# Routing in two interleaved chains, its constants made earlier, and the sixth weight unit's second half loaded later

## The reference

```
1. attention with gates, a recurrence over 768 positions, for 4 batches x 8 heads of width 40:
   C = f*C + i*(v k^T);  y = sigmoid(o) * (C q) / max(|n q|, 1)
2. mixture of 8 experts:  logits = x @ w_gate;  e = argmax(logits)
   out[token] = softmax weight of e * (relu(x @ w1[e]) @ w2[e])
3. dense pair:  h = x @ w_in;  out = max(0.01 h, h) @ w_out
```

## Time and profile before

| | us |
|---|---|
| three runs | 809.02, 803.6, 808.95 |
| median | 808.95 |
| profiled execution, its own time | 808.7 |
| its span, first to last instruction | 807.0 |
| PE busy | 744.9 (92%) |
| DVE busy | 518.1 (64%) |
| ACT busy | 415.4 (51%) |
| POOL busy | 192.6 (24%) |

### The profile page before, as it was taken

One profiled execution on the slowest core, in us unless ns is written; L12 is line 12 of the kernel. 1 busy time (PEld: TensorE's weight loads), 2 busy tenths in 40 slices (PEclk: granted clock), 3 DMA queues, 4 the chain that ended last, 5 costly groups with the idle time before them and its releaser, 6 DMA issues.

```text
span 807.0 us, 17962 instructions
## 1 busy us (share of the span) xinstructions
PE 744.9 (92%) x6435; PEld 551.7 (68%) x6436; DVE 518.1 (64%) x1346; ACT 415.4 (51%) x811; POOL 192.6 (24%) x286
## 2 busy tenths in 40 slices
PE   4899999995488999999999899999999999999994
PEld 3688888885277888888888655556566555565552
DVE  6769898897887457565687565465465455554441
ACT  4578777767753458455664233343433433434332
POOL 4477787874221101111100000020100100100101
PEclk9999999998699999999999999999999999999998
DMA  6879979660527965887220000000000000000000
GB/s 195 221 232 294 326 234 340 184 203 26 176 69 266 358 219 198 262 317 256 84 83 1 2 2 1 0 34 1 25 9 2 32 0 0 32 0 0 34 1 32
DMA packets 39517, 95.87 MB, mean 119 GB/s; under 512 B 7150, under 2 KB 19630, under 8 KB 39438
## 3 DMA queue, kind: packets, MB, share of 16 engines
q1 hardware_dynamic: 31010, 66.33, 26.3%
q10 hardware_dynamic: 5788, 19.47, 6.7%
q0 software_dynamic: 2640, 9.01, 3.4%
HBM read 70.92 MB, written 23.89 MB: 117 GB/s over the span
## 4 chain that ended last, share of the span: by engine, by line
PE 83%; DVE 7%; DMA 3%; issue 3%; ACT 2%; SPq 1%; POOL 1%; ACTq 0%; DVEq 0%; POOLq 0%
PE bank L1694 34%; PE bank L1836 19%; PE bank L1728 12%; PE bank L1557 4%; PE bank L1581 4%; PE bank L1603 1%; PE bank L1684 1%; PE bank L1567 1%; PE bank L1573 1%; DMA slot<-qkT 1%; PE bank L1547 1%; DMA d_x<-og 1%; PE bank L1549 1%; PE bank L1813 1%; ACT slot L787 1%
## 5 line engine op out<-in xcount | busy, mean ns | idle before, releaser
L1694 PE MATMUL bank<-stage,slot 128*128 128x512 f16 x768 | 181.1, 379 | 0.0
L1836 PE MATMUL bank<-slot,dec 128*128 128x320 f16 x768 | 159.1, 299 | 0.0
L1694 PEld LDWEIGHTS bank<-stage,slot 128*128 128x128 f16 x768 | 75.1, 98 | 74.3 <-DVE stage L1489 0.2
L1694 PE MATMUL bank<-qbd,slot 128*128 128x128 f16 x1984 | 117.9, 221 | 7.4 <-issue 6.9
L1694 PEld LDWEIGHTS bank<-qbd,slot 128*128 128x128 f16 x1984 | 113.7, 99 | 11.0 <-issue 10.5
L1493 DVE TENSOR_TENSOR qk<-stage,dec 128x512 f16<-128x512 f32 x96 | 66.4, 692 | 84.7 <-ACT dec L989 84.7
L1836 PE MATMUL bank<-slot,qk 128*128 128x320 f16 x384 | 114.8, 299 | 0.0
L703 POOL DMA_INDIRECT out<-stage,tok_i x24 | 23.6, 983 | 368.6 <-ACT stage L1000 364.7
L989 ACT CAST dec<-stage 128x512 f16<-128x512 f32 x96 | 59.4, 619 | 100.7 <-PE bank L1836 72.0
L1489 DVE TENSOR_TENSOR stage<-bank,stage 128x512 f32<-128x512 f32 x96 | 66.2, 690 | 67.4 <-ACT stage L983 66.9
L983 ACT ACTIVATE stage<-bank 128x512 f32<-128x512 f32 x96 | 57.3, 597 | 97.5 <-PE bank L1694 96.5
(11 more groups left out here) (268 smaller groups left out, 1192.1 us busy)
## 6 DMA issues: line engine op xcount, KB each, us to landing
slot<-d_w SPq DMA_DIRECT2D x12, 1280.0 KB, 6.4
stage<-wB SPq DMA_DIRECT2D x6, 1280.0 KB, 8.3
d_w<-slot ACTq DMA_DIRECT2D x6, 1280.0 KB, 8.3
stage<-wA SPq DMA_DIRECT2D x6, 1024.0 KB, 6.5
d_w<-slot SPq DMA_DIRECT2D x4, 1280.0 KB, 8.7
stage<-wB ACTq DMA_DIRECT2D x4, 1280.0 KB, 9.3
qk<-qkT SPq DMA_DIRECT2D x12, 360.0 KB, 5.7
slot<-qkT SPq DMA_DIRECT2D x12, 360.0 KB, 8.0
```

What stands on the lines that cost most here:

```text
L1694: ins = t_.matmul(pf, a[:, col:col + P], x(k), start=(q == 0), stop=(q == len(ops) - 1))
L1836: ins = t_.matmul(bank[4 + q][:, 0:DM], x[f % 2][:, q * P:(q + 1) * P], slotB[2 + f // NF][:, c0:c0 + DM], start=(f == 0 and z == 0), stop ...
```

## The change

- **Constants earlier.** POOL makes the routing constants (ones, triangle, two index rows, a row of zeros and ones) before its last `gate_one` and `rows`, where it had made them after.
- **Best experts in two parts.** `best(0, 22)` handles steps 0 to 21 before `top(22)`, `scale(4)`, `top(23)`; `best(22, 24)` handles the last two after them. The layout of these matrices on the free axis goes from expert-major to step-major; `oneh` keeps its memory layout and is read and written with a stride of 24 elements.
- **The scan moves ahead of the matmuls.** A running sum over the steps is taken of the one-hots themselves, so PE's three matmuls give the place of each token and the counts directly. Five instructions between the counts and the tile one-hots go.
- **Two chains.** Positions (semaphore `rt`) and expert ends (semaphore `rt_b`) are issued alternately on DVE, each waiting only for its own predecessor.
- **Tiles in two parts.** `bid` is made and multiplied for the first 4 tiles (NX), and for the other 27 after that; `idq` is filled in two parts too.
- **Unit 5.** SP waits for the first two gathers before `load_B(5)`. ACT squares parts 0 and 1 before the first casts, part 2 between `x_high(0)` and `x_high(1)`, parts 3 and 4 after. `sums(5)` goes behind the first two products on PE, `scale(5)` behind `x_scale(3)` on DVE. The highs of unit 5 go one pair later; the lows of units 4 and 5 are spread as the tables below say.
- **WARM** goes from 20 to 12 matmuls, and from 10 to 6. PE reads the experts of pairs 0 and 1 into registers before the first transpose.

```diff
@@ POOL, before the last step's gate
+            pool.wait_ge(pv_done, (NST - 2) * NG)
+            g.memset(onesb, 1.0).then_inc(rt_const, 1)
...
             gate_one(NST - 1, (NST - 1) % NBUF)
             rows(NST - 1, (NST - 1) % NBUF, (NST - 1) % 2)
-            pool.wait_ge(pv_done, NST * NG)
-            g.memset(onesb, 1.0).then_inc(rt_const, 1)
...
@@ SP
             load_A(5)
+            sp.wait_ge(rt_idx, 1)
+            for p in range(2):
+                sp.wait_ge(xt_landed[p], 16)
             load_B(5)
@@ ACT
-            for k in range(NSL):
+            for k in range(2):
                 square(5, k)
...
             x_cast(0, 0)
             x_cast(1, 1)
             x_high(0, 0)
+            square(5, 2)
             x_high(1, 1)
+            for k in range(3, NSL):
+                square(5, k)
             x_cast(2, 0)
@@ DVE
-            top(NST - 2)
-            scale(4)
-            top(NST - 1)
...
+            best(0, NST - 2)
+            top(NST - 2)
+            scale(4)
+            top(NST - 1)
+            dve.wait_ge(lgc_done, NST)
+            best(NST - 2, NST).then_inc(rt_oh, 1)
+            dve.wait_ge(rt_oh, 1)
+            v.tensor_tensor_scan(cum, keep_r, ohf, 0.0, ALU.mult, ALU.add).then_inc(rt_oh, 1)
...
-            rl(v.tensor_reduce(cnt, totals.rearrange("p (e t) -> p e t", e=NE), AX.X, ALU.add))
...
-            rl(v.tensor_tensor_scan(cum, ones_r, totals, 0.0, ALU.mult, ALU.add))
-            ends = cum.rearrange("p (e t) -> p e t", e=NE)[:, :, NST - 1]
-            rl(v.tensor_tensor(delta, past, ends, ALU.subtract))
-            rl(v.tensor_tensor(r1, cum, totals, ALU.subtract))
...
+            rn(v.tensor_tensor(r1, place, first_at.unsqueeze(1).broadcast_to([P, NST, NE]), ALU.add))
+            bn(v.tensor_tensor(past, first_at, cnt, ALU.add))
+            aw()
+            rn(v.tensor_tensor(r1, r1, oneh[:, :, :], ALU.mult))
+            bw()
+            bn(v.tensor_tensor(shift, isk, past.unsqueeze(1).broadcast_to(ee), ALU.mult))
...
+            tiles_of(bid0, 0, NX)
+            marks(bid0)
+            aw()
+            onehots(0, 12)
+            onehots(12, NA)
+            v.tensor_tensor(ohl, iota_j[:, :], plo[:, NST - 1:NST].broadcast_to([P, P]), ALU.is_equal).then_inc(rt_a, 1)
+            tiles_of(bid1, NX, NPAIR)
             dve.wait_ge(rt_id, 1)
-            v.tensor_copy(idq[:, :], bank[6][:, 0:NPAIR]).then_inc(rt_idx, 1)
+            v.tensor_copy(idq[:, 0:NX], bank[6][:, 0:NX]).then_inc(rt_idx, 1)
+            marks(bid1)
...
             x_scale(1, 1)
+            dve.wait_ge(rt_id, 2)
+            v.tensor_copy(idq[:, NX:NPAIR], bank[5][:, 0:NPAIR - NX]).then_inc(rt_idx, 1)
...
             x_low(0, 0)
-            scale(5)
             x_low(1, 1)
...
             x_scale(3, 1)
+            scale(5)
             jobs(0)
@@ PE
-            t_.matmul(psS[0][:, 0:NE * NST], trib, oh, start=True, stop=True)
-            t_.matmul(psS[1][:, 0:NE * NST], onesb, oh, start=True, stop=True).then_inc(rt_cnt, 1)
+            t_.matmul(psS[0][:, 0:RN].rearrange("p (t e) -> p t e", t=NST), trib, oneh[:, :, :], start=True, stop=False)
+            pe.wait_ge(rt_oh, 2)
+            t_.matmul(psS[1][:, 0:NE], onesb, cum.rearrange("p (e t) -> p e t", e=NE)[:, :, NST - 1], start=True, stop=True)
+            t_.matmul(psS[0][:, 0:RN].rearrange("p (t e) -> p t e", t=NST), onesb, cum.rearrange("p (e t) -> p t e", e=NE), start=False, stop=True
+                      ).then_inc(rt_cnt, 1)
...
             pe.wait_ge(rt_tab, 1)
+            now, after = expert(0), expert(1)
             x_turn(0, 0)
-            sums(5)
...
-            h_product(0, 0, expert(0))
-            h_product(1, 1, expert(1))
+            h_product(0, 0, now)
+            h_product(1, 1, after)
+            pe.wait_ge(rt_idx, 2)
+            sums(5)
             pe.wait_ge(rt_bg, 3)
-            pe.wait_ge(sc_chain, scaled(5) - SC_UNIT + 1)
@@ tables
-WARM = 20
+WARM = 12
-PAIR_HI = {0: ((5, 0), (5, 1)), 1: ((5, 2), (5, 3)), 2: ((5, 4),),
+PAIR_HI = {1: ((5, 0), (5, 1)), 2: ((5, 2), (5, 3)), 3: ((5, 4),),
-PAIR_LO = {0: ((4, 0), (4, 1), (4, 2), (4, 3)), 1: ((4, 4), (5, 0)), 2: ((5, 1), (5, 2)), 3: ((5, 3),), 4: ((5, 4),),
+PAIR_LO = {0: ((4, 0), (4, 1), (4, 2)), 1: ((4, 3), (4, 4)), 2: ((5, 0), (5, 1)), 3: ((5, 2), (5, 3)), 4: ((5, 4),),
```

More of the change, by code:

```diff
@@ L1308, in _ @@
[L1308 to L1309 removed]
+            rn(v.tensor_reduce(rank, above, AX.X, ALU.add))
+            bn(v.tensor_tensor(shift, above, cnt.unsqueeze(1).broadcast_to(ee), ALU.mult))
+            aw()
+            rn(v.tensor_tensor(isk, rank.unsqueeze(1).broadcast_to(ee), iota_j[:, 0:NE].unsqueeze(2).broadcast_to(ee), ALU.is_equal))
+            bw()
+            bn(v.tensor_reduce(first_at, shift, AX.X, ALU.add))
```

163 lines of the change are left out of this document (103 added, 60 removed).

## The result

| | kernel before | changed kernel |
|---|---|---|
| median | 807.77 (18 runs) | 811.18 (18 runs) |
| lowest, highest | 803.60, 810.87 | 806.52, 815.43 |
| profiled execution | 808.7, span 807.0 | 810.98, span 808.9 |

The ratio is 1.0043, with a 95% interval of 1.0022 to 1.0063. The change made the kernel 3.4 us slower, where 805.0 was forecast in a range of 800.0 to 808.5. The forecast was wrong in sign and outside its range.

The account below looks back on a forecast made before the run. It took a latency chain of small DVE instructions and gathers before pair 2's product as the bound. That product would start at 233.9 instead of 237.64, so 808.7 - 3.7 = 805.0 us, in a range of 800.0 to 808.5.

Parts of the forecast that it names:

- The failed step: From pair 2's product on: any earlier start moves all that follows equally, if DVE and ACT keep up; 3.7 us.
- so the 3.7 stays: Later pairs: DVE's work of pairs 1 to 3 fits a PE period over 7 us, keeping the 3.7 us gain.
- The stall at 322.63: Rival, PE in pair 13's product: shifted transfers may remove a stop costing 2.1 + 1.6 us, giving 801.2; 18%.
- Best experts in two parts: DVE before the counts: large part hidden, about 2.1 us; six short links remain, -0.86; counts at 197.9 against 198.22.
- Two chains: DVE, counts to first tile comparison: independent instructions overlap, so 4.3 us instead of 7.93.
- First tiles and list: DVE after the chains: 4 tiles take 0.73, then 4.27 to the list, which starts 5.55 us earlier, at 207.2.
- Gathers: After the list: first gather lands near 211.85; DVE's work is last, first tile's scale at 212.3, 5.2 us earlier.
- the 0.4 that I had put against it: First gathers: POOL can't write descriptors during DVE's two-port mode, so gathers and end might slip 0.4 us.
- The load of unit 5: Second half of unit 5's weights: out at 214.0, lands 7.2 later at 221.2, and holds pair 2's product.
- the second term that failed: From unit 5's landing to pair 2's product: 12.7 us, of which 0.4 to get PE's product going after x_low(2).
- PE's own way: PE's path alone: first product at 217.6, pair 2's product at 232.0, 5.6 us earlier, were nothing else late.
- The rival on the clock: Fewer warming matmuls leave PE's first product at 1.2 GHz, 3.75 us more, pair 2's at 235.8, end 806.9; 9%.

Follow-up runs that it names:

- a_pad92: Changed kernel with 92 small unread matmuls added where PE is idle, so the pairs' code lies 255 instructions behind the kernel before; 804.59 us, ratio 0.9958.
- c_best: Changed kernel with one PE loop for pairs 3 to 28, 20 and 10 warming matmuls, top(22) and scale(4) interleaved with best() on DVE; 810.52 us, ratio 1.0024.
- c_best2: Changed kernel with 20 and 10 warming matmuls, top(22) and scale(4) interleaved with best() on DVE, four loops, pairs' code at 255; 806.20 us, ratio 0.9970.
- b_pad36: Kernel before with 36 small unread matmuls added where PE waits, putting the pairs' code 71 instructions later; 813.46 us, ratio 1.0066.

## Why the prediction was wrong

**The failed step** is "whatever starts pair 2's product earlier moves all that follows by as much", and again "so the 3.7 stays". The stretch behind pair 2 was 4.5 us longer in the profiled executions. The runs showed why: the 48 matmuls for the second list, less 12 warming ones, moved PE's code of the pairs by 72 instructions, and the stops of PE that wait for code went from cheap places to dear ones: inside pair 4's product from 0.55 us to 2.39. Moving the kernel before by 71 with empty work costs it 0.66%; moving the changed one on to 255 brings it to 804.59. I had costed the list's second part by its time and counted the warming matmuls by their time, both rightly at nothing, and never by their length in the program.

**The stall at 322.63.** I had seen it and given 18% to its going away, put down to "shifted transfers". It was a stop for code, with its packet at 322.33. In the changed kernel it did go, and 1.25 us ahead of pair 13's product and the stops at pairs 4 and 16 came; in a_pad92 it is there again, 1.37 us long. What I should have asked of that row is what in the change could move it either way, and the answer was on the order of PE's instructions. A stop that can go can also multiply; I had given that side no chance at all.

Point by point, up to pair 2:

- *Best experts in two parts* (forecast -0.86 for the one-hots, measured -0.28: the scan behind them starts at 197.28, where PE's part had been free to start at 197.56). `top(23)` came 0.54 late, and the counts 0.24 late instead of 0.32 early. The large part ran from 191.44 to 194.66, 3.2 us, not 2.1: line 1290 writes the one-hots with a stride, 0.96 us for 176 elements against 0.36 for 192 packed ones, and line 1287 took 0.83 instead of 0.36. I had priced the strided read and forgotten the strided write. `top(22)`, `scale(4)` and `top(23)` stood behind it. The six small links cost 0.22 each (0.21 forecast), and PE's part 0.63 us against 0.66, so its strided read of the scan cost nothing that shows. Why line 1287 is slow isn't settled: it starts 0.08 us behind POOL's gate multiplication at 192.16, which lasts 0.72. The Trainium skill (GPSIMD Engine Reference, Specifications) names a contention of POOL with DVE instructions that have two SBUF inputs; the row agrees. In c_best and c_best2 the comparison starts 0.17 us behind POOL's multiplication instead of 0.08 and takes 0.75 us instead of 0.83: in all kernels with this change it ends about 0.2 us after POOL's does. No run here took POOL's part away.
- *Two chains*: 4.3 forecast, 4.31 measured; the strided multiply took 0.48 against 0.36. The overlap of independent instructions is real.
- *First tiles and list*: 0.73 and 4.27 forecast, 0.99 and 4.19 measured. The list came 4.8 us earlier, not 5.55.
- *Gathers*: the first tile's scale was forecast 5.2 earlier and came 3.65 earlier. DVE was free for it 5.2 us after the list (5.1 forecast); what was late is the gather, for which it waited 0.73, so here the forecast had the wrong one last. POOL took 1.36 us for the issue of the first gather instead of 1.23 and the second went out 1.67 behind it instead of 1.53: beside the second `marks` that is 0.13, not the 0.4 that I had put against it. The transfer itself took the rest. The second gather took 3.47.
- *The load of unit 5*: out at 215.01 (214.0), landed at 220.86 (221.2). `h_low(0)` ended 5.3 us after that, as forecast, and DVE's stretch from there to the end of `x_low(2)` took the forecast 7.0:

```profile
232.61 0.56 DVE L1448 TENSOR_TENSOR qbd<-bank,qbd 128x384 f16<-128x384 f32 x1
```

  That is 226.13 to 233.17. PE's product followed 1.89 us later, not 0.4: 14.2 in all instead of 12.7. This is the second term that failed, and the earlier trace rows had it: `x_low(2)` ended at 235.67, the product started at 237.64, 1.97 apart. In all 17 profiled executions these two are 1.9 to 2.2 us apart; the three transposes of tile 3 (0.5 us) and two reads of an expert's number into a register lie between, and no run took them apart.
- *PE's own way*: first product at 219.25, not 217.6, 1.55 of it from the first tile's scale, which came at 213.86 and not at 212.3. PE had stood idle from 213.70 to 215.99, and the windows behind it show the lower level, 1.2 GHz, for two microseconds and part of the next two (columns as in the earlier trace rows):

```profile
216.00:218.00 2.00, 2.00 (x8) 1.26 (x9) 1.59 (x5) 1.72 (x4) 0.92 (x1) 0.50 0.91 218
218.00:220.00 2.00, 2.00 (x19) 1.68 (x18) 0.11 (x1) 0.98 (x3) 0.98 (x2) 0.65 1.03 411
```

The rival on the clock had the first product itself at half speed, 3.75 us more. It took 3.81 us against 3.75 before: the clock was back 0.1 us behind its start. What ran slow is what stands ahead of it, six warming matmuls in 2.13 us where ten took 1.79 before. And it didn't matter, since the load of unit 5 held pair 2 back longer.

## What to carry to other kernels

Where an engine's program is long and full of jumps, a change moves all code behind it. Before a gain or loss under 1% is put down to what was edited, look for 16 KB packets on the instruction queue beside PE's stops, run the kernel before with as much empty code in an idle place, and the changed kernel padded to the next multiple of 256 instructions: here that alone was worth 5 to 7 us of median, more than the change. And compare stretches between marks, not spans: the end of attention fell anywhere from 189.3 to 194.3 us in these profiled executions, whatever the kernel.

## What the runs showed of the hardware

- PE stopped inside a product without a semaphore where the code crossed a certain place: 0.3 to 2.6 us up to 34 matmuls behind the jump, 0.2 to 0.8 us 55 to 62 matmuls into a straight body. The place repeats after 255 or 256 instructions of PE. In all 24 such stops PE went on 2.26 to 2.77 us after a 16 KB packet of instructions had started, so the stop is short where the packet starts early. Of the 20 such packets between pair 2 and pair 29 in the changed kernel most cost nothing. What starts a packet stays open: the stops at pairs 4, 13 and 16 don't lie whole multiples of 256 built instructions apart.
- A stop can cost twice. After PE stood still for about 2 us the next product often took 5.37 us instead of 3.75. The changed kernel's window behind such a stop has a granted clock of 0.72, between the levels of 1.2 and 2.4 GHz:

```profile
349.00:355.00 6.00, 6.00 (x71) 5.77 (x71) 0.74 (x2) 1.28 (x3) 0.00 (x0) 0.72 0.37 154
```

  In b_pad36 that was pair 3 (2.13 us of standing), while in the changed kernel pair 3 stood for 2.00 and took 3.74.
- A strided write of 176 16-bit elements took DVE 0.95 to 0.96 us in all kernels with the change, the packed one of 192 took 0.36; one operand is also repeated along another axis there, but the subtraction ahead of it, with the same repetition and a packed result, took 0.40.
- A comparison and branch in PE's loop cost about 0.10 us each (1.86 us over 12 pairs with 18 of them), although PE's matmuls run one after the other there.
